# Block means of V by column-tiled matmuls, in a fused attention, gated-MLP and LayerNorm-MLP kernel

## The reference

```python
k_sum = k.reshape(B, H, nb, block, D).max(axis=3)      # block = 32, nb = 24
v_sum = v.reshape(B, H, nb, block, D).mean(axis=3)
scores_l = scale * q @ k.T ; mask_l = abs(i - j) < 16
scores_s = scale * q @ k_sum.T + log(block)
a = softmax(concat([where(mask_l, scores_l, -1e9), scores_s]))
out = a @ concat([v, v_sum])
```

## Time and profile before

| | |
|---|---|
| median of 3 runs | 481.77 us |
| profiled execution | 482.58 us |
| its span (first to last instruction) | 480.9 us |
| TensorE matmuls busy | 466.8 us, 97% |
| VectorE busy | 289.0 us, 60% |
| ScalarE busy | 211.7 us, 44% |
| GpSimd busy | 265.3 us, 55% |
| HBM read | 31.08 MB |

### The profile page before, as it was taken

How to read it: one execution, slowest core, us unless ns; L and a number is a source line. 1 busy time by engine, 2 the same in 40 slices (tenths; PEclk the granted TensorE clock), 3 DMA queues, 4 the chain that set the end, 5 groups by cost and what they waited for, 6 DMA issues and landing times.

```text
span 480.9 us, 7972 instructions
## 1 busy us (share of the span) xinstructions
PE 466.8 (97%) x2807; PEld 416.4 (87%) x2807; DVE 289.0 (60%) x621; ACT 211.7 (44%) x517; POOL 265.3 (55%) x409
## 2 busy tenths in 40 slices
PE   7998889999999999999999999999999999999997
PEld 7886677899998988988898889899988999899985
DVE  6998887578755795995663364267564243333333
ACT  3888788744333665634533423333401332233110
POOL 3546788999900500028788886892006378778100
PEclk9999999999999999999999999999999999999999
DMA  9997992121100200000221022112020112211003
GB/s 211 242 231 187 230 230 78 46 89 44 45 0 1 88 1 0 1 0 1 88 89 59 29 89 89 47 42 87 2 109 23 34 55 87 89 46 44 0 1 131
DMA packets 62115, 35.63 MB, mean 74 GB/s; under 512 B 48064, under 2 KB 55004, under 8 KB 61788
## 3 DMA queue, kind: packets, MB, share of 16 engines
q1 hardware_dynamic: 60508, 34.72, 26.4%
q10 hardware_dynamic: 1568, 0.39, 0.4%
HBM read 31.08 MB, written 3.15 MB: 71 GB/s over the span
## 4 chain that ended last, share of the span: by engine, by line
PE 84%; SPq 5%; DVE 4%; POOL 2%; issue 2%; ACT 1%; DMA 1%; DVEq 0%; POOLq 0%; ACTq 0%
PE two L1407 9%; PE two L1406 9%; PE two L1405 9%; PE two L1382 8%; PE two L1385 8%; PE two L1384 8%; PE two L1244 5%; PE two L1246 5%; PE two L1245 5%; PE two L1312 5%; PE two L1313 5%; PE two L1311 5%; SPq L366 2%; PE two L1195 1%; PE two L1329 1%
## 5 line engine op out<-in xcount | busy, mean ns | idle before, releaser
L1382 PE MATMUL two<-combo,wa 128*128 128x384 f32 x224 | 75.8, 338 | 0.1
L1407 PE MATMUL two<-wv,h 128*128 128x512 f32 x192 | 75.4, 393 | 0.0
L1385 PE MATMUL two<-combo,wa 128*128 128x384 f32 x224 | 75.4, 337 | 0.0
L1406 PE MATMUL two<-wv,h 128*128 128x512 f32 x192 | 75.3, 392 | 0.0
L1384 PE MATMUL two<-combo,wa 128*128 128x384 f32 x224 | 75.2, 336 | 0.0
L1405 PE MATMUL two<-wv,h 128*128 128x512 f32 x192 | 75.0, 391 | 0.0
L555 POOL TENSOR_TENSOR asum<-wst 128x256 f32<-128x256 f32 x26 | 22.7, 873 | 93.7 <-PE two L1246 50.2
L584 POOL TENSOR_TENSOR wa<-wst,wa 128x256 fp32r<-128x256 f32 x39 | 29.6, 789 | 40.9 <-ACT wa L1028 40.9
L549 POOL TENSOR_TENSOR wa<-asum,wa 128x256 fp32r<-128x256 f32 x52 | 43.8, 843 | 4.3
L518 POOL TENSOR_SCALAR pn<-ex,rinv 128x120 f32<-128x120 f32 x96 | 33.5, 368 | 21.7 <-DVE rinv L654 21.7
L1056 ACT ACTIVATE h<-u 128x384 fp32r<-128x384 f32 x32 | 16.8, 526 | 61.6 <-DVE u L858 53.8
(11 more groups left out here) (117 smaller groups left out, 1029.5 us busy)
## 6 DMA issues: line engine op xcount, KB each, us to landing
wst<-in_moe_w_ch SPq DMA_DIRECT2D x26, 512.0 KB, 3.4
vW<-in_v SPq DMA_DIRECT2D x16, 240.0 KB
kn<-in_k SPq DMA_DIRECT2D x15, 192.0 KB, 3.7
qn<-in_q SPq DMA_DIRECT2D x15, 192.0 KB, 4.0
out<-y SPq DMA_DIRECT2D x11, 256.0 KB, 2.0
vblk<-in_v SPq DMA_DIRECT2D x3, 768.0 KB, 6.7
wst<-in_moe_w_in SPq DMA_DIRECT2D x8, 256.0 KB, 3.5
wst<-in_moe_w_out SPq DMA_DIRECT2D x8, 256.0 KB, 2.8
```

The source lines that it names most:

```text
L1382: nc.tensor.matmul(o, wk[:, 0, kk], ck[:, 0, kk], start=(first and kk == 0), stop=False, skip_group_check=True)
L1385: ins = nc.tensor.matmul(o, wk[:, 1, kk], ck[:, 0, kk], start=False, stop=(kk == 1), skip_group_check=True)
L1406: nc.tensor.matmul(o, hi, vl, start=False, stop=False, skip_group_check=True)
L1407: ins = nc.tensor.matmul(o, lo, vh, start=False, stop=(f == NFP - 1 and c == 1), skip_group_check=True)
```

## The change

`block_means(p)` now makes the means for all 8 pairs. The 12 matmuls of a pair (one for each query block b = 3g + a) go in four column groups: g gives the PSUM partitions 32g to 32g + 31, and a the place in an accumulation of three. The `means` matrix gets wider, so that a shifted slice of 32 columns puts each result into the right rows. VectorE copies the 128x128 result once (`means_out`, new) to `vs`, and SyncE's queue spreads it into `vW` with two DMAs a pair, each 12 source rows times 12 query blocks of 128 floats. The second load of V, `block_sums`, their semaphores and their buffers are gone.

`block_means(p-1)` stands in `keys_t(p)` for p from 3 on, ahead of the transposes and behind the waits; that of pair 7 stands ahead of the 28-row transpose in step 18. On VectorE the last step of a pair becomes `score_max`, `row_sums`, `key_max`, `means_out`, `x_low`, `window_keys`; before it was `score_max`, `key_max`, `x_low`, `row_sums`, `window_keys`. The orders of the first five steps are written anew on VectorE, ScalarE and TensorE. On SyncE the means' loads wait for `vm_done`, and the weight loads move.

```diff
-        SUMS = {3: ((1, 0),), 4: ((1, 1),), 7: ((2, 0),), 9: ((2, 1),), 12: ((3, 0),), 15: ((3, 1),)}
-        vblk = at("vblk", [4 * NB, BLK, D], F32)
+        vs = at("vs", [P, 2, P], F32)
-        means = at("means", [KEYS, 2 * NB - 2], F32)
+        means = at("means", [KEYS, 2 * MC + 2], F32)      # MC = 30
+        def means_at(p):
+            if p < 2:
+                return ps_o[p][:, GT:GT + P]
+            return ps_kq[:, 0:P] if p < NPAIR - 1 else ps_kq[:, TOK0:TOK0 + P]
# SyncE
             def load_vsum(p):
-                sp.wait_ge(vsum_done, p // 2)
-                c = p % 2
-                for h in range(2):
-                    src = vs[NB * (2 * c + h):NB * (2 * c + h + 1), p // 2 % 2]
-                    sp.dma_start(vW[p % 3][KEYS:KW, :, D * h:D * (h + 1)],
-                                 src[:, None, :].broadcast_to([NB, NQ, D])).then_inc(v_in[p % 3], 16)
+                sp.wait_ge(vm_done, p + 1)
+                for u in range(2):
+                    src = vs[26 + D * u:26 + NB // 2 + D * u, p % 2]
+                    sp.dma_start(vW[p % 3][KEYS + NB // 2 * u:KEYS + NB // 2 * (u + 1)],
+                                 src[:, None, :].broadcast_to([NB // 2, NQ, P])).then_inc(v_in[p % 3], 16)
...
             load_q(2)
-            load_vblk(1)
+            load_vsum(0)
             load_k(3)
+            load_v(2)
+            load_vsum(1)
+            load_w(0)
             load_q(3)
-            load_v(2)
-            load_w(0)
...
-                if p == 4:
-                    load_vblk(3)
-                if p == 2:
-                    load_vsum(p)
-                    load_vblk(2)
                 if p + 1 < NPAIR:
                     load_v(p + 1)
-                if p != 2:
-                    load_vsum(p)
-                for n in {3: (1,), 4: (2,), 5: (3,), 7: (4,)}.get(p, ()):
+                load_vsum(p)
+                for n in {2: (1,), 4: (2,), 5: (3,), 6: (4,)}.get(p, ()):
                     load_w(n)
# VectorE
+            def means_out(p):
+                dve.wait_ge(vm_ready, p + 1)
+                if p >= 2:
+                    dve.wait_ge(v_in[(p - 2) % 3], v_loads(p - 2))
+                nc.vector.tensor_copy(vs[:, p % 2], means_at(p)).then_inc(vm_done, 1)
...
             score_max(0)
+            key_max(1)
             score_max(1)
-            key_max(1)
             row_sums(0)
+            window_keys(1)
             score_max(2)
+            means_out(0)
             row_sums(1)
-            window_keys(1)
-            row_sums(2)
-            dve.wait_ge(vm_ready, 1)
-            nc.vector.tensor_copy(vW[0][KEYS:KW], means_of(0)).then_inc(vm_done, 1)
             key_max(2)
             score_max(3)
+            row_sums(2)
+            score_max(4)
+            means_out(1)
             window_keys(2)
-            for n in range(3, NG):
+            row_sums(3)
+            for n in range(4, NG):
                 p, t = n // GPP, n % GPP
-                if n == 3:
-                    row_sums(n)
                 if n + 1 < NG:
                     score_max(n + 1)
                 if t == 2 and p + 2 < NPAIR:
+                    row_sums(n)
                     key_max(p + 2)
-                x_low(n - 3)
-                if n > 3:
-                    row_sums(n)
+                    means_out(p + 1)
+                if n == 4:
+                    row_sums(4)
+                    x_low(0)
+                elif n == 5:
+                    x_low(1)
+                    x_low(2)
+                else:
+                    x_low(n - 3)
+                    if t != 2 or p + 2 >= NPAIR:
+                        row_sums(n)
                 if t == 2 and p + 2 < NPAIR:
                     window_keys(p + 2)
-                for it, half in SUMS.get(n, ()):
-                    block_sums(it, half)
                 if n == COLS_STEP + 1:
                     dve.wait_ge(cols_ready, 1)
+                    means_out(NPAIR - 1)
# ScalarE
             exps(1)
+            queries(1)
             exps(2)
-            queries(1)
             probs_out(0)
+            exps(3)
             probs_out(1)
-            for n in range(3, NG):
+            exps(4)
+            x_high(0)
+            probs_out(2)
+            queries(2)
+            x_high(1)
+            probs_out(3)
+            for n in range(5, NG):
                 p, t = n // GPP, n % GPP
                 exps(n)
-                if n == 3:
-                    x_high(0)
-                if n == 4:
-                    act.wait_ge(vm_ready, 2)
-                    nc.scalar.copy(vW[1][KEYS:KW], means_of(1)).then_inc(vm_done, 1)
+                if n == 5:
+                    x_high(2)
# TensorE
+            def block_means(p):
+                pe.wait_ge(v_in[p % 3], v_windows_in(p))
+                if p < 2:
+                    pe.wait_ge(means_done, 1)
+                    pe.wait_ge(q_done, p + 1)
+                for a in range(3):
+                    for g in range(4):
+                        c = MC - 2 * a - (26 if g % 2 == 0 else 0)
+                        ins = nc.tensor.matmul(means_at(p)[32 * g:32 * (g + 1)], means[:, c:c + 32], vW[p % 3][0:KEYS, 3 * g + a],
+                                               start=(a == 0), stop=(a == 2), skip_group_check=True)
+                ins.then_inc(vm_ready, 1)
...
                 if p >= 3:
                     pe.wait_ge(q_done, p)
+                if p >= 3:
+                    block_means(p - 1)
                 transposes(kn[:, p % 2], ps_kq, ktr_ready)
...
             scores(0)
+            keys_t(1)
             scores(1)
-            keys_t(1)
+            queries_t(1)
             scores(2)
-            queries_t(1)
             block_means(0)
+            keys_t(2)
             probs_t(0)
-            keys_t(2)
             scores(3)
+            scores(4)
+            block_means(1)
             probs_t(1)
-            scores(4)
             outputs(0)
             outputs(1)
             for n in range(3, NG):
                 p, t = n // GPP, n % GPP
                 probs_t(n - 1)
+                if n == 3:
+                    scores(5)
                 if t == 0 and p < NPAIR - 1:
                     queries_t(p + 1)
-                if n + 2 < NG:
+                if n > 3 and n + 2 < NG:
                     scores(n + 2)
-                if n == 3:
-                    block_means(1)
```

More of the change, by code:

```diff
@@ L44, in conv_gated_attention_kernel @@
     EPS = 1e-6
+    MC = 30
     assert D == 64 and DM == 512 and T == 6 and KW == 120 and FF == 1024 and GPP == 3
@@ L105, in conv_gated_attention_kernel @@
         ks = at("ks", [P, NB], F32)
-        vs = at("vs", [4 * NB, 2, D], F32)
         st = at("st", [P, NTT, 6], F32)
@@ L123, in conv_gated_attention_kernel @@
         qn = at("qn", [P, 2, T, 2, D], F32)
-        vblk = at("vblk", [4 * NB, BLK, D], F32)
-        vW = [at(f"vW{i}", [P, NQ, P], F32) for i in range(2)]
-        vW.append(None)
+        vs = at("vs", [P, 2, P], F32)
+        VW_AT = place[0] + 7168
+        vW = [at("vW0", [P, NQ, P], F32, VW_AT), at("vW1", [P, NQ, P], F32), None]
         sm = at("sm", [P, 2, GB, KW], F32)
@@ L193, in conv_gated_attention_kernel @@
         q_first = sem("q_first")
-        vblk_in = sem("vblk_in")
         w_in_sem = [sem("w_in0"), sem("w_in1")]
@@ L204, in conv_gated_attention_kernel @@
         xh_done, x_done = sem("xh_done"), sem("x_done")
-        vsum_raw, vsum_done = sem("vsum_raw"), sem("vsum_done")
         h_ready, h_done, t0_done = sem("h_ready"), sem("h_done"), sem("t0_done")
@@ L220, in conv_gated_attention_kernel, with v_windows_in @@
         o_dma = sem("o_dma")
-        v_blocks = v.rearrange("b h (n i) d -> (b h n) i d", i=BLK)
         out_rows = out.rearrange("b s d -> (b s) d")
         w1_cols = w_ch1.rearrange("(c p) f -> p c f", p=P)
+        def v_windows_in(p):
+            return 16 * (6 * (p // 3) + 4)
         def v_loads(p):
-            return 16 * sum(4 if i < 2 else 6 for i in range(p % 3, p + 1, 3))
+            return 16 * 6 * (p // 3 + 1)
         TOK0 = P
@@ L247, in v_windows @@
             return bass.AP(a.tensor, a.offset, [[D, nw], [QB * D, nb], [1, D]])
-        def means_of(p):
-            return ps_o[0][KEYS:KW, None, 0:P].broadcast_to([NB, NQ, P])
+        def means_at(p):
+            if p < 2:
+                return ps_o[p][:, GT:GT + P]
+            return ps_kq[:, 0:P] if p < NPAIR - 1 else ps_kq[:, TOK0:TOK0 + P]
         def x_parts(n):
@@ L349, in load_q @@
                                  q[b, 2 * hp + h].rearrange("(t p) d -> p t d", p=P)).then_inc(qn_in[p % 2], 16)
[L351 to L355, removed]
             def load_v(p):
@@ L487, in _ @@
             link(nc.gpsimd.memset(means[:], 0.0))
-            link(nc.gpsimd.memset(means[:, NB - 2:NB], 1.0 / BLK))
-            link(nc.gpsimd.affine_select(out=means[:, NB - 2:NB], in_=means[:, NB - 2:NB], compare_op=ALU.is_ge, fill=0.0,
```

(20 more changed lines are left out.)

## The result

| | before | after |
|---|---|---|
| median in one comparison, 15 runs each | 483.68 us (481.33 to 485.14) | 480.39 us (480.17 to 482.64) |
| ratio | 1 | 0.9942 [0.9926, 0.9957] |
| profiled execution | 482.58 us, span 480.9 | 480.42 us, span 478.7 |
| HBM read | 31.08 MB | 28.72 MB |

The changed kernel is faster by 0.6%. The two profiled executions differ by 2.2 us, the ratio stands for 2.8 us and the medians are 3.3 us apart: before's runs scatter over nearly 4 us and its profile is one of the better ones, while 13 of the 15 runs after lie between 480.2 and 480.9. Why, the experiments show further down. The forecast time, 480.4, was built on before's first three runs (481.77), so that it met the median is luck. The forecast gain was 1.4 us. Measured are 2.2 between the two profiles, from whose rows it was built, and 2.8 by the ratio of all runs, twice the forecast.

What follows compares the result with a forecast made beforehand. A loop between engines, or the DMA, was taken to pace the first 80 us. Gains 1.55 (start) + 0.1 (four pairs) - 0.25 (end) = 1.4 us, so 481.77 - 1.4 = 480.4 us; 8-in-10 range 476.5 to 484.2.

Steps and rivals of the forecast that it cites:

- The bound: First 80 us: a loop between engines (ScalarE's P copies transposed probabilities, Q makes queries) or the DMA sets the pace.
- The means: Middle step, TensorE's path: 24 records take 0.93 us (0.70 to 2.8); P waits 1.18 instead of 0.27, pair 10.31.
- The first five steps: Step 4's exps, E(4), at 20.0 instead of 24.41; pair 3's queries at 32.8 instead of 34.36: 1.55 us gained.
- End of attention: block_means(7) before the 28-row transpose: P of step 18 waits some 0.2 us more; 0.25 us lost in the sum.
- The spread of the means: DMA spread on SyncE's queue lands at 6.1 us, outputs need it at 7.4: hidden, with 1.3 us of slack.
- The load: Three second V loads of 768 KB removed; GpSimd's 3.8 us on `w_in`, which make the 2.16 us wait, go.
- The order and the sums on VectorE: P's second wait goes; sums cost within 1.51 us a pair; with the load, these give what the means take.
- (a): Rival: the means hide in TensorE's waits; a pair takes 9.1 us, the kernel 475.2, or 477.8 for half; chance 0.21.
- (b): Rival: V comes late for the means, TensorE stands 3.8 us once; kernel 484.2 us; chance 0.13.
- (c): Rival: the means' column groups don't overlap; 1.9 us more in six pairs, 11 us; kernel 491.8; chance 0.05.
- (d): Rival: array drains before and after the means, two 0.27 us latencies, 3.2 us in six pairs; 483.6 us; chance 0.07.
- (e): Rival: the early lead isn't there, a DMA or semaphore holds steps 3 to 5; kernel 482 us; chance 0.08.

Runs made afterwards that it cites:

- means_twice: The changed kernel with the 12 matmuls of block_means issued twice for pairs 2 to 7: 483.44 us, ratio 1.0009 to before.
- old_start: The changed kernel with the first five steps in before's order on TensorE, VectorE and ScalarE, SyncE's queue unchanged: 486.39 us, ratio 1.0062 to before.
- short_sums_load: The kernel before with block sums over 2 of 32 rows and the second V loads cut to those rows: 479.89 us, ratio 0.9921.
- short_sums: The kernel before with block sums over 2 of the 32 rows, loads and order as before: 484.13 us, ratio 1.0011.
- sums_first: The kernel before with VectorE's row_sums ahead of key_max in a pair's last step: 483.43 us, ratio 1.0.
- w_early: The kernel before with the second chunk of w_in loaded one pair earlier, as in the changed kernel: 484.56 us, ratio 1.0023.
- means_gap: The changed kernel with block_means of pairs 2 to 6 in the pair's first step, between probability and query transposes: 479.15 us, ratio 0.9905 to before.

## Why the prediction was right, by its steps

**The bound.** Right. The loop of TensorE and ScalarE sets the pace; the 0.66 us that means_twice put into TensorE's part came out in P's wait, and 0.49 of it in the pair.

**The means.** Right in place and mechanism, a little large in size: 0.93 us taken (24 times the unrounded spacing of 0.0381 is 0.91), 0.79 measured, between the lower bound of 0.70 and the value taken. The outputs' spacing was the right row to lean on. P of the middle step waits 1.06 to 1.15 (1.18), Q 0.28 to 0.49 (0.3), the pair takes 10.27 (10.31). Four pairs gained 41.37 - 41.07 = 0.3 (0.1).

**The first five steps.** E(4) 20.05 (20.0), Q(2) 23.05 (23.35), P(4) 28.72 (29.0), Q of pair 3 at 32.45 (32.8): 1.91 gained (1.55). Together 2.2 at Q of pair 7 (1.65), and the span is shorter by 2.2. What was wrong in this step is its meaning: I took it for a gain that stands by itself, and old_start shows it as a condition of the new queue order.

**End of attention.** Not confirmed: 0.25 us of loss were taken, and the 2.2 us by which Q of pair 7 is ahead are still 2.2 at the end of the span.

**The spread of the means.** "1.3 us of slack" was wrong. The chain of waits after, by start and duration:

```profile
41.39 0.80 SPq L365
42.19 0.04 issue
42.23 0.44 SPq L366
42.67 0.04 issue
42.72 0.81 SPq L374
43.53 0.05 issue
43.58 2.97 DMA vW<-vs
46.55 0.18 issue
46.73 0.69 PE two L1227 x16
```

The copy was done at 40.08, but SP came to the spread at 42.72, behind V's loads, and it landed at 46.55; P (46.04 + 0.69 for the way to the outputs) wanted it at 46.73: 0.2 us. I had counted the issues of the spread and of a whole pair, and not the entries of the queue just ahead of it.

**The load.** The stall on `w_in` goes, as predicted. Its 1.4 us were in the sum, since they are in before's average pair of 10.34: the four pairs took 10.46, 11.12, 10.07 and 9.72 us, and short_sums_load brings all four to 9.71. Between the two profiles 2.2 us were measured and not 1.4 by the sum of small differences above: 0.36 more at the start, 0.2 more in the four pairs, and 0.25 not lost at the end.

The load has its part in the rest, from 2.2 between the profiles to 2.8 and 3.3 between all runs. Here my sum had no term: for the halved clock behind the stall, in executions where TensorE stands a little longer. In short_sums the clock is 0.20, 0.50 and 0.16 short of full in the three stretches of 2 us from 50 to 56 us; that makes 1.7 us of 481.5, which is the whole of its mean of 0.996. Before's times in the three later sets go with that mean: at 1.0 they are 481.4 to 483.6 us (one of 1171 us left out), at 0.996 483.0 to 484.7, at 0.993 484.2 to 485.7. Of the 15 runs after, two had 0.996, and these took 482.4 and 482.6. The profile that I read was at 1.0 throughout. At 1.0 before's medians are 482.4 to 483.1 and after's 480.4, so of the 3.3 us between the medians the clock accounts for 0.6 to 1.3. That is a reading of run averages, with the stretch itself seen in short_sums, sums_first, w_early and old_start; no trace of before at 0.996 was kept.

**The order and the sums on VectorE.** In the whole each alone gained nothing (ratios 1.0 and 1.0011). What I wrote, that load, sums and order give what the means take, holds, but the load decides whether the rest counts. short_sums takes 0.8 us out of the pair from Q at 34.33 (9.70 for 10.46), with the load still there, and loses it at the stall; only short_sums_load, 3.8 us below before, keeps it. How the 3.8 us divide between load and sums isn't shown beyond that.

**The rivals.** (a) fell: nothing took the means up; moved to a better place (means_gap) a pair still takes 9.90, not 9.1. (b) fell: no wait was for V. The waits of pairs 2 and 3 for `vW<-vs` held the outputs by under 0.1 us each, against P's start + 0.69. (c) fell: 0.0275 us a record. The Trainium skill ("TensorE: Matmul & The Clock Gate", Part 3, the mechanism) lets a weight load overlap only across row groups; here all loads use the same rows, other columns, and the measured number decides against it: in after four weight loads start at 37.13 to 37.15 us, while the first four matmuls, started at 37.10 to 37.12 and 0.3 us long, are running. (d) fell in size: from the start of the means to the start of the key transposes is 0.79 us, and their records overlap by 0.86 - 0.79. But a change of shape isn't free. From the last record of the means to the first transpose it is 0.20 us, from the outputs to the means 0.15, where groups of transposes follow each other at 0.11: 0.04 to 0.09 us a change, and not 0.27. (e) fell: the lead was 4.36 us.

**Left open.** old_start with the spread later in the queue wasn't tried. Full sums with the short load wasn't tried, so the sums' cost in an uncrowded queue isn't known. Nor was it tried whether the second load crowded the queue by its bytes or by its packets.

## What to carry to other kernels

When a queue is full, the stall that the profile names is only the entry that happened to be late: moving it moves the stall, and the gain lies in taking transfers out. Recomputing on an engine what would be loaded again can pay even on the critical path, if the work is spread over four column groups in turn. In a queue that issues in order, an entry that waits for a result holds everything behind it, so the result has to be ready when the queue comes to it. And when an addition goes into a loop of two engines, price the path by the distance from each group's start to the next one's: that gave the wait to 0.1 us here.

## What the runs showed of the hardware

- Small float32 matmuls with 128 moving columns and 32 weight columns: 0.117 us a record in one column group, 0.0275 in four taken in turn (the second 24 records of means_twice), 0.066 when three matmuls (six records) follow each other in one group (1.59 us for 24).
- A change of shape among 128x128 transposes, outputs in two column groups and means in four took 0.15 to 0.20 us from start to start, where groups of transposes follow each other at 0.11.
- After TensorE had stood 1.5 to 3 us in a stretch already thin in work, the granted clock was at or near the 1.2 GHz level for 2 to 4 us in five traces (0.50 in short_sums from 52 to 54 us, 0.64 in w_early from 60 to 64). It isn't so behind each such stand: in old_start the 1.63 us before 41.95 left the clock at 1.00, as did the 1.06 us before 51.34 in the kernel before. Where it falls, a stall costs more than its own length.
- A broadcast of 72 KB from SBUF to SBUF (half of a pair's spread) landed 3.0 us after its issue; the wait for its turn in the queue was nearly as long (40.08 to 42.72).
